# An attention, MLP and experts kernel: requests, score banks and the first steps put in another order

## What is computed

```python
# attention, 4 batches, 8 heads, 576 tokens, head dimension 64, window 128
scores = q @ k.T / 8;  scores += -slope[h] * |rel|;  masked to 0 <= rel < 128
attn = softmax(scores);  x = attn @ v            # as 2304 tokens x 512
# MLP, 512 -> 2048 -> 512
h = x @ w_in;  y = (h * clip(h + 3, 0, 6) / 6) @ w_out
# router and 8 experts, 512 -> 1024 -> 512, one expert for each token
e = argmax(cosine(y, expert_emb) / tau)
out = gate * (relu(y @ w1[e]) @ w2[e])
```

## Time and profile before

| what | us |
|---|---|
| median of 3 runs (lowest, highest) | 850.04 (849.13, 850.17) |
| the profiled execution, its own time | 849.08 |
| span in its trace | 847.4 |
| PE busy in the span | 823.6 |
| DVE, ACT, POOL busy | 478.2, 395.5, 242.8 |

### The profile page before, as it was taken

How to read it: one execution, slowest core, us unless ns; L and a number is a source line. 1 busy time by engine, 2 the same in 40 slices (tenths; PEclk the granted TensorE clock), 3 DMA queues, 4 the chain that set the end, 5 groups by cost and what they waited for, 6 DMA issues and landing times.

```text
span 847.4 us, 18689 instructions
## 1 busy us (share of the span) xinstructions
PE 823.6 (97%) x6508; PEld 705.6 (83%) x6508; DVE 478.2 (56%) x1469; ACT 395.5 (47%) x1056; POOL 242.8 (29%) x262
## 2 busy tenths in 40 slices
PE   5899999999999999999999999999999999999996
PEld 4788888888888888888888888878888888888885
DVE  6655576665666666656665578766553435554000
ACT  4655555454555455454454436534343434333342
POOL 5984000000000000000000101277666556666432
PEclk9999999999999999999999999999999999999999
DMA  8665311112111021121000016474455534542100
GB/s 227 191 175 161 111 51 46 32 38 72 43 51 58 19 64 50 52 76 32 21 27 1 27 31 194 152 260 153 149 162 172 154 138 139 156 151 75 45 18 11
DMA packets 54428, 80.20 MB, mean 95 GB/s; under 512 B 11752, under 2 KB 28136, under 8 KB 54210
## 3 DMA queue, kind: packets, MB, share of 16 engines
q1 hardware_dynamic: 50050, 67.58, 26.2%
q0 software_dynamic: 4000, 11.29, 4.1%
q10 hardware_dynamic: 288, 0.13, 0.1%
HBM read 69.51 MB, written 11.30 MB: 95 GB/s over the span
## 4 chain that ended last, share of the span: by engine, by line
PE 91%; DVE 3%; DMA 2%; ACT 2%; SPq 1%; issue 1%; POOL 0%; POOLq 0%; ACTq 0%; DVEq 0%
PE ps_h L810 23%; PE ps_y L825 22%; PE ps_h L943 16%; PE ps_s L982 15%; PE ps_out L764 3%; PE ps_s L727 3%; PE ps_y L967 3%; PE ps_out L982 1%; PE ps_out L912 1%; DMA y_scratch<-gate_tok 1%; PE ps_s L746 1%; PE ps_s L752 1%; DMA arena<-in_k 1%; PE ps_s L749 1%; ACT gated_hi L1088 0%
## 5 line engine op out<-in xcount | busy, mean ns | idle before, releaser
L810 PE MATMUL ps_h<-x_hi,win_hi 128*128 128x256 f32 x576 | 170.1, 295 | 5.3 <-DVE x_lo L1323 2.8
L810 PE MATMUL ps_h<-x_hi,win_lo 128*128 128x256 f32 x576 | 162.9, 283 | 0.0
L810 PE MATMUL ps_h<-x_lo,win_hi 128*128 128x256 f32 x576 | 162.7, 282 | 0.0
L1349 DVE TENSOR_TENSOR gated_lo<-gated,gated_hi 128x256 fp32r<-128x256 f32 x144 | 65.4, 454 | 103.2 <-ACT gated_hi L1088 103.2
L810 PEld LDWEIGHTS ps_h<-x_hi,win_hi 128*128 128x128 f32 x576 | 109.6, 190 | 14.2 <-DVE x_lo L1323 3.9
L1088 ACT CAST gated_hi<-gated 128x256 fp32r<-128x256 f32 x144 | 58.5, 406 | 133.9 <-PE ps_y L825 100.6
L825 PE MATMUL ps_y<-wout_hi,gated_hi 128*128 128x512 f32 x288 | 114.0, 396 | 0.2 <-DVE gated_lo L1349 0.2
L599 POOL MEMSET arena<- 128x64 bf16 x2 | 0.2, 151 | 396.4 <-DVE x_lo L1323 396.4
L825 PE MATMUL ps_y<-wout_hi,gated_lo 128*128 128x512 f32 x288 | 113.8, 395 | 0.0
L825 PE MATMUL ps_y<-wout_lo,gated_hi 128*128 128x512 f32 x288 | 112.1, 389 | 0.0
L810 PEld LDWEIGHTS ps_h<-x_lo,win_hi 128*128 128x128 f32 x576 | 109.8, 191 | 2.4
(11 more groups left out here) (228 smaller groups left out, 1559.4 us busy)
## 6 DMA issues: line engine op xcount, KB each, us to landing
arena<-in_moe_w SPq DMA_DIRECT2D x64, 512.0 KB, 4.6
arena<-in_v SPq DMA_DIRECT2D x40, 128.0 KB, 3.2
y_scratch<-y_sb SPq DMA_DIRECT2D x9, 512.0 KB, 3.9
arena<-in_v SPq DMA_DIRECT2D x16, 256.0 KB, 3.3
en_all<-in_moe_w_in SPq DMA_DIRECT2D x16, 256.0 KB, 4.0
en_all<-in_moe_w_out SPq DMA_DIRECT2D x16, 256.0 KB, 3.0
arena<-in_q SPq DMA_DIRECT2D x31, 128.0 KB, 2.6
arena<-in_k SPq DMA_DIRECT2D x31, 128.0 KB, 3.0
```

The lines of the kernel that those rows point to most:

```text
L810: last = pe.matmul(ps_h[m % 2][:, 0:TB], a[:, c, w], r[:, c, x], start=n == 0, stop=n == 3 * KC - 1)
L1349: dve.tensor_tensor(gl[m % 2][:], gate[:], gh[m % 2][:], ALU.subtract).then_inc(dve_gl, 1)
```

## The change

1. **Requests.** SP asks for q and k of steps 1, 2 and 3 before anything else, then for piece 0, v of group 0, pieces 1 to 3 and v of group 1. The ring of weight buffers has 6 places instead of 4 (`WR`), the two new ones in memory that the biases' distances used, so SP waits once for `dve_before`. v of group 2 is asked for in iteration 3 instead of 1, the row of zeros in iteration 4, and v of every later group one iteration later than before: group 3 in iteration 6, behind that iteration's pieces of the weights.
2. **Banks.** Scores of steps 1 and 3 go to `ps_y`, so scores of steps 2 and 3 come one behind the other on PE, ahead of transposes of step 0. Values of step 0 come after transposes of step 1, scores of step 4 after transposes of step 2.
3. **DVE's first steps.** Biases for the keys before go behind scores of step 0 and of step 1; `take_x` of steps 0 and 1 goes around `normalise(2)`.
4. **A block's first slot.** `up` waits for x_hi first and takes its eight products with x_hi before it waits for x_lo.
5. **Embeddings.** ACT's square and root of the expert embeddings (L1184, L1186), with the loads of its tables, go from iteration 4 to iterations 6 and 7; DVE's part and the store follow in iteration 8.
6. **Router.** The dot products are spread over one slot less, so that the last slot of a block has none.

```diff
-    EMB_AT, EN_AT = FIRST - 1, FIRST + 4
+    EMB_AT, EN_AT = FIRST + 2, FIRST + 4
+    WR = 6
+    AHEAD_OF = (4, 4, 6, 8, 10, 12)
...
+        def scored_in(s):
+            return ps_y if s < EARLY and s % 2 else ps_s
...
             def fetch_w(n):
-                reach(sp, pool_wl, n - 3)
-                sp.dma_start(w_raw[n % 4], w_piece(n)).then_inc(ld_w[n % 4], 16)
+                reach(sp, pool_wl, n + 1 - WR)
+                sp.dma_start(w_raw[n % WR], w_piece(n)).then_inc(ld_w[n % WR], 16)
...
-            start_at_one(sp, counting)
             load_qk(1)
-            load_v(0)
             load_qk(2)
+            start_at_one(sp, counting)
+            load_qk(3)
             for n in range(4):
                 sp.dma_start(w_raw[n], w_piece(n)).then_inc(ld_w[n], 16)
-            sp.wait_ge(pool_z, 3)
-            sp.dma_start(y_dram[0:1, :], zero_row).then_inc(st_zero, 16)
+                if n == 0:
+                    load_v(0)
             load_v(1)
...
-                    for n in range(FIRST + 5, ALONE + 4):
+                    for n in range(AHEAD_OF[it], ALONE + WR):
                         fetch_w(n)
...
-                        if n + 4 < W_PIECES:
-                            fetch_w(n + 4)
-                            fetch_w(n + 5)
+                        if n + WR < W_PIECES:
+                            fetch_w(n + WR)
+                            fetch_w(n + WR + 1)
...
-                    if NQ * (g - 1) - 1 + OUT == it:
+                    if NQ * (g - 1) + OUT == it:
                         load_v(g)
...
-                reach(pe, dve_s, 4 * s)
+                reach(pe, dve_s, 4 * (s if s > EARLY else s - 1))
...
             def up(m):
-                    pe.wait_ge(dve_xl, last_step(blk) + 1)
+                    s = last_step(blk)
+                    if s < EARLY:
+                        pe.wait_ge(dve_xh, s + 1)
+                    else:
+                        pe.wait_ge(act_xh, s + 1 - EARLY)
...
+                kinds = ((win_h, xh), (win_l, xh), (win_h, xl))
+                order = [(c, kind) for c in range(KC) for kind in kinds]
+                if f == 0:
+                    order = [(c, kind) for kind in kinds for c in range(KC)]
+                for n, (c, (a, r)) in enumerate(order):
+                    if f == 0 and n == 2 * KC:
+                        pe.wait_ge(dve_xl, last_step(blk) + 1)
...
                 if it == 1:
                     scores(2)
-                elif 2 < it < STEPS:
+                    scores(3)
+                elif FIRST <= it < STEPS:
                     scores(it)
...
-                if OUT <= it < FIRST:
+                if 2 < it < FIRST:
                     values(it - OUT)
                 if 0 <= it - 1 < STEPS:
                     transposes(it - 1)
+                if it == 2:
+                    values(0)
+                if it == 3:
+                    scores(4)
...
-                if it == EMB_AT:
+                for m in mine[2:]:
+                    slot(m)
+                if it == EMB_AT - 1:
                     act.wait_ge(ld_emb, 16)
                     act.activation(emb_sq, emb_rows, ACT.Square, accum_out=st[:, 0:1]).then_inc(act_emb, 1)
+                if it == EMB_AT:
                     act.wait_ge(act_emb, 1)
                     act.activation(st[:, 1:2], st[:, 0:1], ACT.Sqrt).then_inc(act_emb, 1)
-                for m in mine[2:]:
-                    slot(m)
...
-                    late, span = (2, FC - LAG - 3) if blk == 1 else (0, FC - LAG - 1)
+                    late, span = (2, FC - LAG - 4) if blk == 1 else (0, FC - LAG - 2)
```

More of the change, by code:

```diff
@@ L278, in _program @@
         zero_row = y[0:1, :, :].rearrange("p a n -> p (a n)")[:, 0:W]
-        w_raw = [en[:, 4 + i, :] for i in range(4)]
+        w_raw = [en[:, (4 + i) % E, :] for i in range(WR)]
         flat = en[:].rearrange("p e d -> p (e d)")
@@ L327, in _program @@
         ld_v = [sem(f"ld_v{i}") for i in range(3)]
-        ld_w = [sem(f"ld_w{i}") for i in range(4)]
+        ld_w = [sem(f"ld_w{i}") for i in range(WR)]
         st_zero, st_en, st_y = sem("st_zero"), sem("st_en"), sem("st_y")
@@ L552, in split_w @@
                 if n < ALONE or n % 2:
[L553 to L554 removed]
+                    pool.wait_ge(ld_w[n % WR], 16 * (n // WR + 1))
+                    pool.tensor_copy(hi, w_raw[n % WR]).then_inc(pool_wh, 1)
                     pool.wait_ge(pool_wh, min(n, ALONE) + max(n - ALONE, 0) // 2 + 1)
@@ L557, in split_w @@
                     pool.wait_ge(act_wh, (n - ALONE) // 2 + 1)
-                pool.tensor_tensor(lo, w_raw[n % 4], hi, ALU.subtract).then_inc(pool_wl, 1)
+                pool.tensor_tensor(lo, w_raw[n % WR], hi, ALU.subtract).then_inc(pool_wl, 1)
             pool.iota(rel_i, pattern=[[1, TB]], base=-P, channel_multiplier=-1).then_inc(pool_m, 1)
@@ L726, in scores @@
                             keys = kT[d, 2 * q4 + j, :, :].rearrange("p a r -> p (a r)")[:, key:key + n]
-                            last = pe.matmul(ps_s[hh][HP * h:HP * (h + 1), U * j + at:U * j + at + n],
+                            last = pe.matmul(scored_in(s)[hh][HP * h:HP * (h + 1), U * j + at:U * j + at + n],
                                              qT[s % 3][d, j, HP * h:HP * (h + 1)], keys, start=True, stop=True)
@@ L806, in up @@
                 w, x = slice(f * P, (f + 1) * P), slice(blk * TB % RING, blk * TB % RING + TB)
[L807 to L812, removed]
+                kinds = ((win_h, xh), (win_l, xh), (win_h, xl))
[5 more added lines that the diff above has]
+                        pe.wait_ge(dve_xl, last_step(blk) + 1)
+                    last = pe.matmul(ps_h[m % 2][:, 0:TB], a[:, c, w], r[:, c, x],
+                                     start=n == 0, stop=n == 3 * KC - 1)
                 last.then_inc(pe_h, 1)
@@ L816, in down @@
                 blk, f = divmod(m, FC)
+                if m == 0:
+                    pe.wait_ge(dve_s, 4 * EARLY)
                 if f == 0:
@@ L1118, in split_high @@
                 for n in split_by_act(m):
-                    act.wait_ge(ld_w[n % 4], 16 * (n // 4 + 1))
-                    act.copy(next(iter(w_split(n))), w_raw[n % 4]).then_inc(act_wh, 1)
+                    act.wait_ge(ld_w[n % WR], 16 * (n // WR + 1))
+                    act.copy(next(iter(w_split(n))), w_raw[n % WR]).then_inc(act_wh, 1)
             def take_yT(n):
@@ L1279, in scores @@
                     j, hh = divmod(n, 2)
-                    scored, biases = ps_s[hh][0:R, U * j:U * (j + 1)], bias[0:R, 4 * q4 + n, 0:U]
+                    scored, biases = scored_in(s)[hh][0:R, U * j:U * (j + 1)], bias[0:R, 4 * q4 + n, 0:U]
                     if i == 0:
@@ L1585, in _ @@
                     take_x(it - OUT)
-                elif 1 < it <= FIRST or FIRST < it <= STEPS and len(slots(it - 1)) < 2:
+                elif it in (2, FIRST) or FIRST < it <= STEPS and len(slots(it - 1)) < 2:
                     normalise(it - 1)
@@ L1590, in _ @@
                     bias_own()
-                    bias_before(0, 4)
                 if it < STEPS:
                     scores(it)
-                if OUT <= it < STEPS + OUT and not x_first and it != FIRST - 1:
+                if it == 0:
+                    bias_before(0, 4)
+                if it == 1:
+                    bias_before(4, H)
+                    normalise(0)
+                if it == 3:
+                    take_x(0)
+                    normalise(2)
+                    take_x(1)
+                if FIRST <= it < STEPS + OUT and not x_first:
                     take_x(it - OUT)
-                if it == 0:
-                    bias_before(4, H)
-                if it == 1:
-                    normalise(0)
                 if it == EMB_AT + 1:
```

17 lines of the change are left out of this document (10 added, 7 removed).

## The result

The changed kernel takes 850.91 us (median of 17 runs, 849.99 to 852.8), the kernel before 849.54 us (17 runs beside them, 848.08 to 851.31). The ratio is 1.0015 with a 95% interval of 1.0008 to 1.0021: 0.7 to 1.8 us slower, and still inside the 0.2% that I had set as "no change". The time lies in the range of the prediction, but on the wrong side of zero: it is what rival (a) gave (850.9), not the forecast (848.8). That 850.9 fits so closely is in part luck: rival (a) was 0.9 us above the 850.04 of the prediction, and the measured difference is 1.4 us, above a median that came out 0.5 us lower. The profiled execution took 850.99 us, its span is 849.3 against 847.4 us.

What follows compares the result with a forecast made beforehand. PE bounds the kernel, busy 823.6 of 847.4 us. Step 6 starting 1.3 us later less 2.46 at block starts gave -1.2: 847.9 us profiled, 848.8 against the median; own range 846.5 to 851, with (a) and (c) 846.0 to 852.3.

Steps and rivals of the forecast that it cites:

- rival (a): At values of step 6, the clock falls in the stall and costs 2.1 us more: 850.9 us; chance 0.33.
- v of group 3: Before values of step 6, PE waits 5.1 us for this load, starting at 62.4, 1.3 us later than before.
- The sum: Whole kernel: 1.3 us later at step 6, 2.46 won at block starts, -1.2 us, clock kept; chance 0.45.
- (b): At step 6, v is in time and every gain is kept, 6.3 us: 843.8 us; chance 0.08.
- The landing: Third load of v of group 3 lands 3.5 us after its issue; the skill's 2.0 us was set aside.
- The first steps: Before step 6: heads give 1.1 us and later table loads 1.3, together 2.4, between 0 and 3.6.
- The ring of six: Iteration 7: two more weight buffers remove PE's waits for gated and gated_lo, gain 1.42 us, other end 0.
- Tables later: Table loads moved to iterations 6 and 7 remove PE's wait for gated of slot 0, gain 1.3 us, other end nothing.
- Block starts and router: At four block starts after 60 us, all 2.46 us of waits for x_lo go, other end 1.5.
- rival (c): Denser dot products or later tables cost as much as the block starts give: 851.2 us; chance 0.07.
- one after 70 us that was not there before: Sign that the prediction is wrong: PE has waits after 70 us that were not there; no size given.
- From 60 us on, whatever PE is late or early is kept to the end: From 60 us to the end, PE's lead or delay carries through; only 2.5 us of waits for x_lo there.

Runs made afterwards that it cites:

- v3_first: The changed kernel with only v of group 3 asked for ahead of the weight pieces, still in iteration 6: 846.96 us, ratio 0.9921 to the kernel before.
- v_late_alone: The kernel before with only v of group 3 and later groups asked for one iteration later: 858.67 us, ratio 1.0073.
- warm_stall: The changed kernel with 19 extra matmuls, results overwritten, on PE ahead of values of step 6: 852.93 us, ratio 0.9996 to the kernel before.
- v_early: The changed kernel with v of group 3 and later asked for in the iteration of before (group 3 in 5): 848.73 us, ratio 0.9944 to the kernel before.
- all_but_heads: The kernel before with ring of six, block starts, router and later tables, without the new first steps, v of group 3 as before: 848.57 us, ratio 0.9945.
- both: all_but_heads with the store of the gates behind two loads of the experts' weights instead of five: 849.02 us, ratio 0.9952 to the kernel before.
- ring_six: The kernel before with only the ring of six weight buffers, v of group 3 still in iteration 5: 851.57 us, ratio 0.9968.
- tables_later: The kernel before with only the embeddings' square, root and table loads moved to iterations 6 and 7, DVE's part to 8: 855.5 us, ratio 1.0007.
- block_starts: The kernel before with only up waiting for x_hi first and the router's dot products over one slot less: 850.91 us, ratio 0.9966.
- changed_again: The changed kernel itself, unaltered, measured against the kernel before in another session: 854.95 us, ratio 1.0018.
- gates_ahead: v3_first with the store of the gates behind two loads of the experts' weights instead of five: 849.36 us, ratio 0.9954 to the kernel before.

## Where the prediction was right and where it was wrong

**v of group 3: right.** I gave piece 25 done at 57.0, v landed and values of step 6 at 62.4. Measured: piece 25 is the first of the two at 56.36, which take 2.54 together, so it was done near 57.6; SP issued v at 58.07 and values started at 62.72. The terms behind it held too: POOL started at 9.83 (I took 9.5) and waited 1.00 us for piece 1 (0.8). The stall was 4.42 us where I had 5.1, because PE was less early than I thought. `v3_first` and `v_late_alone` show that the queue position is the cause.

**The step that failed.** "The sum. +1.3 - 2.46 = -1.2 us": it holds a stall at an unchanged clock, the case to which I gave 0.45. The term for the clock was put at nothing. The clock fell, and that cost 2.52 us (`warm_stall` shows it by holding the clock); with this term the same sum is +1.4 us, which is what the runs differ by. That it fits so well is in part luck: with the 0.3 us by which v came later than I took, the 0.71 us at the tokens and the 0.5 us won back the trace makes +1.9, while the medians differ by 1.4. I had rival (a) with its place and a price of 2.1, and gave it 0.33 only. The row for it was there: the earlier trace rows had the clock falling within some 3 us of the last matmul, at the end of the same trace. I discounted it because it stood at the end and not between matmuls, though nothing in the trace gave a reason for such a difference. The Trainium skill, TensorE: Matmul & The Clock Gate, HAM oscillation, describes it: in its example a wait for a DMA between matmuls, several microseconds long, sends the array back to half clock, and the work behind it starts cold. By that rule the forecast had to be (a), and the trace agrees: 0.50 in the window from 62, and 1.76 us instead of 1.08 for 32 matmuls. It agrees again in `v_late_alone` and at the gathered tokens of `v_early`. Not every wait does it: behind the 1.78 us of `warm_stall` the clock stayed at 1.00.

One of the sums on the chances was wrong too: (b) with 0.08 and a third of 0.45 make 0.23 for "faster", not 0.28.

**The landing.** I took 3.5 us from the rows; measured 3.6 for the last load. The 2.0 us of the Trainium skill, DMA: Bandwidth & Descriptors, Anatomy of one DMA, would have been 1.6 us short.

**The first steps: right place, size off.** I took 2.4 us by the start of step 6 from the heads and tables. Values of step 4 start at 33.38 against 34.21 before, a gain of 0.83, and up of slot 0 even starts later (26.28 against 25.96, where I had 24 to 25.5); up of slot 2 starts at 30.39 (28 to 30). The clock again has a part in it. PE's timeline, the changed kernel:

```profile
19.68 1.76 PE L778 MATMUL ps_out<-arena 128*64 128x64 f32 x32
...
23.31 1.76 PE L778 MATMUL ps_out<-arena 128*64 128x64 f32 x32 [0.40 <-ACT arena L1091]
...
33.38 1.08 PE L778 MATMUL ps_out<-arena 128*64 128x64 f32 x32
```

and `v_early`, whose code is the same to here:

```profile
19.38 1.76 PE L778 MATMUL ps_out<-arena 128*64 128x64 f32 x32
...
23.00 1.08 PE L778 MATMUL ps_out<-arena 128*64 128x64 f32 x32 [0.41 <-ACT arena L1091]
...
32.09 1.08 PE L778 MATMUL ps_out<-arena 128*64 128x64 f32 x32
```

In `v_early` values of step 3 run at full pace and in the changed kernel they do not: the granted clock rose between the two groups in the one and only in the window from 27 us in the other. From 23.31 to 33.38 are 10.07 us, from 23.00 to 32.09 are 9.09. So 1.0 us of the head's gain hangs on when the clock rises, and it came out differently in executions of one code: values of step 4 start anywhere from 31.61 to 33.55 in seven traces with the same heads. Without the heads, but with the later tables and the block starts, they start at 33.94 (`all_but_heads`) and 32.85 (`both`), and at 34.21 before. So the 2.4 us lie inside the spread of single executions, and no run shows that the heads give them.

**The ring of six: right, and more.** I gave 1.42, other end 0. `ring_six` shows 1.95 at values of step 6. In the changed kernel PE was ready for them at 58.30 against 61.12, 2.8 us where I had 3.8: 1.6 less up to values of step 4, and 0.6 more from there on.

**Tables later: right only beside the ring.** The 1.3 us were counted as a gain of their own. Alone they turn into a wait for POOL (`tables_later`). Beside the ring most of them stay: in `both` values of step 3 start at 23.55, as in `ring_six` (23.58), and values of step 6 at 58.09 against 59.17, 1.08 us earlier, of which 0.34 are the wait for x_lo before slot 0.

**Block starts and router: right.** 2.46 us predicted, 2.40 measured in `block_starts` on PE's idle time; rival (c) is out.

**Rival (b): its size was right, its condition was not met.** With v in time I had 6.3 us. `v_early`, where it is met, has a lead of 6.0 us at the gathered tokens in the trace, and ratios that make 4.8 us (`v_early`) and 6.7 us (`v3_first`) of 849.54. v's place in the queue stood between the change and this, and at the end of the MLP the gathered tokens.

**What I did not see.** In the trace of before PE reached the gathered tokens at 527.06 and they had landed at 527.01: no wait, so no row in the list of waits, but no slack either. The store ahead of them takes longer in every other trace (10.1 us and more against 9.4). Where its place in the queue is the old one, PE waits 0.7 to 3.7 us, with a fall of the clock in the seven traces in which it waits about 3 us or more. I had named such a wait, one after 70 us that was not there before, as a sign that the prediction is wrong, and the 0.71 us are one. "From 60 us on, whatever PE is late or early is kept to the end" held for PE's own lead; it left out a chain that moves with PE but whose length is not constant.

**What stays open.** Why 3.4 us pass between the small packets of the store and its landing in one execution and over 7 in another, whether the changed kernel or the chip has any part in that, and how to have the store early without delaying the weights. Whether `v3_first` beats `v_early` is not resolved, as their intervals overlap. Both beat the kernel before, and by their ratios the changed kernel.

## What to carry to other kernels

A request in a queue inherits every wait ahead of it: before moving a load behind others, look up what the last of these waits for and when that is done. A stall of PE amid dense matmuls costs its length and, in the stalls of 3 us and more here, 1.3 to 2.5 us of half clock on top, so price it with the clock's rows, also where they stand elsewhere in the trace. And look for transfers that land just as their reader arrives: they are in no list of waits, and any execution in which they are slower shows on the engine that bounds the kernel.

## What the runs showed of the hardware

From 56 us on, the granted clock fell with every wait of PE between matmuls of 2.98 us or more: the three for v (4.42 us in the changed kernel, 5.81 in `v_late_alone`, 6.26 in `changed_again`) and the seven for the tokens (2.98 to 3.70 us). In four of these seven it fell only when PE was already at work again, up to 1 us after. It did not fall in the stretch of 1.78 us in `warm_stall`, where filler matmuls had covered the rest, nor with the 2.24 us in `gates_ahead`. It was not back at once: in the changed kernel dense matmuls ran at 0.50 from 62.72 into the window from 68.

The price beyond the stall does not follow the stall's length: 2.52 us for 4.42, 1.44 for 5.81, 1.32 for 6.26. It follows the time for which PE worked at 0.50: 5.8, 3.3 and 3.1 us, so 0.43 us for each. At the tokens of `v_early` it was 1.56 us.

An 8 KB store of the gates took 9.4 to 13.5 us from issue to landing. In `v_early`, issued at 505.11 and landed at 517.24, the DMA engines carried few bytes in the second of these stretches:

```profile
505.00:510.00 5.00, 5.00 (x40) 4.52 (x39) 3.92 (x19) 3.20 (x6) 0.00 (x0) 1.00 1.02 257
510.00:515.00 5.00, 5.00 (x34) 4.53 (x33) 3.29 (x10) 3.05 (x6) 0.00 (x0) 1.00 0.15 3
```

In `both`, with two loads ahead of it instead of five, its packets moved within 2.5 us and it landed after 10.1. So its slowness is not only a matter of the loads ahead of it, and bytes say little of its time. Whether single elements of 4 bytes are the reason was not tried.
